# Another hand-written order of four engines around the chunks of a scan that runs beside an MLP

## The reference

```python
mag = np.sqrt(a_re * a_re + a_im * a_im)
scale = np.minimum(mag, 0.999) / (mag + 1e-06)
for t in range(S):
    new_re = ar * S_re - ai * S_im
    new_im = ar * S_im + ai * S_re
    S_re, S_im = (new_re + k[t] outer v[t], new_im)
    y[t] = q[t] @ S_re
h = y @ w_in;  x = (h * clip(h + 3, 0, 6) / 6) @ w_out
h = x @ w2_in; out = (max(h, 0) + alpha * min(h, 0)) @ w2_out
```

## Time and profile before

| | before |
|---|---|
| runs, median (lowest to highest) | 1002.93 us (1001.9 to 1004.77), 3 runs |
| the profiled execution | 1003.23 us |
| its span, first to last instruction | 1001.5 us |
| mean granted clock of PE | 0.998 |
| busy PE, DVE, ACT, POOL | 96%, 58%, 50%, 27% |

### The profile page before, as it was taken

How to read it: one execution, slowest core, us unless ns; L and a number is a source line. 1 busy time by engine, 2 the same in 40 slices (tenths; PEclk the granted TensorE clock), 3 DMA queues, 4 the chain that set the end, 5 groups by cost and what they waited for, 6 DMA issues and landing times.

```text
span 1001.5 us, 17747 instructions
## 1 busy us (share of the span) xinstructions
PE 964.9 (96%) x6858; PEld 868.4 (87%) x6858; DVE 584.1 (58%) x1049; ACT 502.0 (50%) x907; POOL 268.2 (27%) x251
## 2 busy tenths in 40 slices
PE   2899989999999999999999999999999999999998
PEld 2788978999999999999999998888888888888786
DVE  6868886777777767777662345444434444344332
ACT  7767886777777777776643543322222122222111
POOL 0000222222232322322222333332333333323332
PEclk9999999999999999999999999999999999999999
DMA  7853334333444333444320801023060060230000
GB/s 218 216 151 95 96 86 109 94 98 80 111 101 126 95 97 80 108 108 111 88 49 1 308 1 56 0 74 85 1 151 8 0 158 1 68 91 1 32 0 32
DMA packets 86661, 84.72 MB, mean 85 GB/s; under 512 B 31152, under 2 KB 81328, under 8 KB 86192
## 3 DMA queue, kind: packets, MB, share of 16 engines
q1 hardware_dynamic: 86576, 83.58, 31.3%
HBM read 55.10 MB, written 14.19 MB: 69 GB/s over the span
## 4 chain that ended last, share of the span: by engine, by line
PE 82%; ACT 5%; DVE 4%; SPq 3%; DMA 2%; issue 2%; ACTq 0%; DVEq 0%
PE op L1263 12%; PE hp L1264 12%; PE op L1264 11%; PE hp L1263 11%; PE op L1265 11%; PE hp L1265 11%; PE yp L1251 3%; PE gp L1258 2%; PE gp L1230 2%; PE yp L1230 2%; PE hp L1286 2%; PE op L1311 2%; DMA a_sb<-a_in 1%; DMA st<-rows 1%; ACT L608 1%
## 5 line engine op out<-in xcount | busy, mean ns | idle before, releaser
L584 POOL TENSOR_TENSOR g_lo<-gated,g_hi 128x512 fp32r<-128x512 f32 (+2 forms) x240 | 266.0, 1108 | 726.2 <-ACT g_hi L679 726.2
L679 ACT ACTIVATE g_hi<-gated 128x512 fp32r<-128x512 f32 (+2 forms) x240 | 126.3, 526 | 314.7 <-DVE gated L969 273.7
L965 DVE TENSOR_SCALAR gate<-hp,alpha_sb 128x512 f32<-128x512 f32 x96 | 72.0, 750 | 209.5 <-PE hp L1265 209.5
L954 DVE SCALAR_TENSOR_TENSOR gated<-gate,hp 128x256 f32<-128x256 f32 (+1 forms) x160 | 75.2, 470 | 134.1 <-ACT gate L672 133.5
L1263 PE MATMUL op<-g_hi,wb_hi 128*128 128x256 f32 (+1 forms) x432 | 137.5, 318 | 2.3 <-ACT out_sb L684 1.2
L1263 PE MATMUL hp<-x_hi,wa_hi 128*128 128x256 f32 (+1 forms) x432 | 134.8, 312 | 0.3 <-DVE x_lo L918 0.2
L1265 PE MATMUL op<-g_hi,wb_lo 128*128 128x256 f32 (+1 forms) x432 | 132.4, 306 | 0.0
L1264 PE MATMUL hp<-x_lo,wa_hi 128*128 128x256 f32 (+1 forms) x432 | 132.3, 306 | 0.0
L1265 PE MATMUL hp<-x_hi,wa_lo 128*128 128x256 f32 (+1 forms) x432 | 132.3, 306 | 0.0
L1264 PE MATMUL op<-g_lo,wb_hi 128*128 128x256 f32 (+1 forms) x432 | 132.3, 306 | 0.0
L672 ACT ACTIVATE gate<-hp,half 128x256 f32<-128x256 f32 (+1 forms) x160 | 81.2, 507 | 98.7 <-PE hp L1265 89.2
(11 more groups left out here) (115 smaller groups left out, 1652.7 us busy)
## 6 DMA issues: line engine op xcount, KB each, us to landing
st<-prod SPq DMA_DIRECT2D x96, 145.1 KB, 3.0
raw<-a_in SPq DMA_DIRECT2D x4, 2304.0 KB, 15.2
a_sb<-a_in SPq DMA_DIRECT2D x24, 288.0 KB, 3.7
qk_sb<-qk_in SPq DMA_DIRECT2D x24, 288.0 KB, 3.7
rows<-prod SPq DMA_DIRECT2D x48, 96.8 KB, 2.4
st<-rows SPq DMA_DIRECT2D x48, 96.8 KB, 2.8
v_pad<-v_in SPq DMA_DIRECT2D x24, 192.0 KB, 3.5
x_raw<-x SPq DMA_DIRECT2D x6, 768.0 KB, 16.2
```

The costliest lines, as they stand in the source:

```text
L584: pool.tensor_tensor(g_lo[:, at, 0:wide], gated[:, at * UT:at * UT + wide], g_hi[:, at, 0:wide].bitcast(F32), ALU.subtract).then_inc(glo_d ...
L679: act.activation(g_hi[:, at, 0:wide], gated[:, at * UT:at * UT + wide], ACT.Copy).then_inc(ghi_done, 1)
L954: dve.scalar_tensor_tensor(out=gated[:, to], in0=gate[:, at], scalar=1.0, in1=hp[:, n % 2, 0:wide], op0=ALU.min, op1=ALU.mult).then_inc(ga ...
L965: dve.tensor_scalar(gate[:, at], hp[:, n % 2, 0:wide], 0.0, alpha_sb[:, m:m + 1], ALU.min, ALU.mult).then_inc(gate_done, 1)
```

## The change

The strings and `places()` go. Each engine gets a `short_slot` and a `long_slot` in which every step stands where it is to be issued; items over 7 (short) or 5 (long) follow with their own steps only. `due` leaves a step out where there is no such chunk, `if_kept` for a batch's last chunk. `ALONE` and `LENGTHS` differ. A few waits are added that the former order made needless. (SP's calls of `store_due` for the last items of a slot are left out below.)

```diff
-ALONE = 3
-LENGTHS = (6,) + 8 * (7,) + (8, 7, 7, 8) + 2 * (5, 5, 6) + (5, 6, 6)
+PLANNED = {True: 7, False: 5}
+ALONE = 2
+LENGTHS = 6 * (7,) + (8, 7, 7, 8, 8, 7, 7) + 4 * (5,) + (6, 5, 6, 5, 6)
...
@@ SyncE's queue
+    def short_slot(n, c0, c1, c2, c4):
+        due(stack, c1)
+        store_due(n)
+        due(stack_high, c1)
+        due(load_v, c1)
+        store_due(n + 1)
+        due(load_qk, c2)
+        due(load_a, c4)
+        store_due(n + 2)
+    def long_slot(n, c0, c1, c2, c4):
+        due(stack, c1)
+        store_due(n)
+        due(load_qk, c2)
+        due(stack_high, c1)
+        store_due(n + 1)
+        store_due(n + 2)
+        due(load_v, c1)
+        due(load_a, c4)
...
@@ ScalarE
+    def short_slot(n, c0, c1, c2, c3):
+        splits(n)
+        gate_of(n + GSTEP)
+        if_kept(copy_k, c0, 0)
+        high_due(n + GSTEP)
+        leave_due(n)
+        splits(n + 1)
+        gate_of(n + 1 + GSTEP)
+        due(waves, c1)
+        due(copy_ends, c1)
+        if_kept(copy_k, c0, 1)
+        high_due(n + 1 + GSTEP)
+        leave_due(n + 1)
+        splits(n + 2)
+        gate_of(n + 2 + GSTEP)
+        due(logs, c2)
+        high_due(n + 2 + GSTEP)
+        leave_due(n + 2)
+        splits(n + 3)
+        gate_of(n + 3 + GSTEP)
+        due(inverses, c2)
+        high_due(n + 3 + GSTEP)
+        x_high(c0)
+        leave_due(n + 3)
+        splits(n + 4)
+        gate_of(n + 4 + GSTEP)
+        high_due(n + 4 + GSTEP)
+        leave_due(n + 4)
+        splits(n + 5)
+        gate_of(n + 5 + GSTEP)
+        due(squares, c3)
+        high_due(n + 5 + GSTEP)
+        leave_due(n + 5)
+        splits(n + 6)
+        gate_of(n + 6 + GSTEP)
+        due(angle, c2)
+        high_due(n + 6 + GSTEP)
+        leave_due(n + 6)
+    def long_slot(n, c0, c1, c2, c3):
+        gate_of(n + GSTEP)
+        if_kept(copy_k, c0, 0)
+        high_due(n + GSTEP)
+        leave_due(n)
+        gate_of(n + 1 + GSTEP)
+        due(copy_ends, c1)
+        due(waves, c1)
+        due(logs, c2)
+        high_due(n + 1 + GSTEP)
+        leave_due(n + 1)
+        due(squares, c3)
+        x_high(c0)
+        gate_of(n + 2 + GSTEP)
+        due(inverses, c2)
+        high_due(n + 2 + GSTEP)
+        leave_due(n + 2)
+        gate_of(n + 3 + GSTEP)
+        if_kept(copy_k, c0, 1)
+        high_due(n + 3 + GSTEP)
+        leave_due(n + 3)
+        gate_of(n + 4 + GSTEP)
+        due(angle, c2)
+        high_due(n + 4 + GSTEP)
+        leave_due(n + 4)
...
@@ VectorE
     def state(c):
...
+            dve.wait_ge(y_ready, c + 1)
             dve.tensor_tensor(win(s_pad), s_sum[:, :, :], ends, ALU.mult).then_inc(state_ready, 1)
...
+    def short_slot(n, c0, c1, c2, c3):
+        due(phases, c1)
+        gate1(n + GSTEP)
+        due(fractions, c1)
+        mask(c0, 0)
+        splits(n)
+        gate1(n + 1 + GSTEP)
+        due(backward, c1)
+        mask(c0, 1)
+        due(with_qk, c1)
+        splits(n + 1)
+        gate1(n + 2 + GSTEP)
+        due(product, c1, 0)
+        splits(n + 2)
+        due(product, c1, 1)
+        gate1(n + 3 + GSTEP)
+        due(decays, c2)
+        x_low(c0)
+        splits(n + 3)
+        if_kept(state, c0)
+        gate1(n + 4 + GSTEP)
+        due(residue, c2)
+        due(refine, c2)
+        due(ratio, c2)
+        splits(n + 4)
+        gate1(n + 5 + GSTEP)
+        due(mags, c3)
+        splits(n + 5)
+        gate1(n + 6 + GSTEP)
+        due(forward, c2)
+        splits(n + 6)
+    def long_slot(n, c0, c1, c2, c3, led):
+        if not led:
+            due(forward, c1)
+        due(phases, c1)
+        mask(c0, 0)
+        gate1(n + GSTEP)
+        due(fractions, c1)
+        due(backward, c1)
+        mask(c0, 1)
+        gate1(n + 1 + GSTEP)
+        due(with_qk, c1)
+        due(product, c1, 0)
+        due(product, c1, 1)
+        gate1(n + 2 + GSTEP)
+        x_low(c0)
+        gate1(n + 3 + GSTEP)
+        due(residue, c2)
+        due(refine, c2)
+        due(ratio, c2)
+        due(mags, c3)
+        gate1(n + 4 + GSTEP)
+        due(decays, c2)
+        if_kept(state, c0)
...
@@ TensorE
     def turn_k(c, k):
...
+        pe.wait_ge(st_landed[c % 2], 16 * ROWS_DMAS * (c // 2 + 1))
         need(pe, tp_read, 2 * kept(c) + k)
...
     def new_state(c):
         pe.wait_ge(tp_read, 2 * kept(c) + 2)
+        pe.wait_ge(v_landed, 16 * (c + 1))
+        pe.wait_ge(masked, 2 * c + 1)
...
-    for steps, n, c0, c1, c2, c3 in places():
-        keeps = not is_last(c0)
-        if "a" in steps:
-            score(c0, 0)
-            if keeps:
-                turn_k(c0, 0)
-        first_half(n)
-        if "a" in steps:
-            score(c0, 1)
-        second_half(n)
-        if "a" in steps and keeps:
-            turn_k(c0, 1)
-        if "o" in steps:
-            outputs(c0)
-            if keeps:
-                new_state(c0)
+    def short_slot(n, c0):
+        first_half(n)
+        score(c0, 0)
+        if_kept(turn_k, c0, 0)
+        score(c0, 1)
+        second_half(n)
+        if_kept(turn_k, c0, 1)
+        first_half(n + 1)
+        second_half(n + 1)
+        first_half(n + 2)
+        second_half(n + 2)
+        first_half(n + 3)
+        outputs(c0)
+        if_kept(new_state, c0)
+        second_half(n + 3)
+        first_half(n + 4)
+        second_half(n + 4)
+        first_half(n + 5)
+        second_half(n + 5)
+        first_half(n + 6)
+        second_half(n + 6)
+    def long_slot(n, c0):
+        score(c0, 0)
+        if_kept(turn_k, c0, 0)
+        first_half(n)
+        if_kept(turn_k, c0, 1)
+        second_half(n)
+        first_half(n + 1)
+        score(c0, 1)
+        second_half(n + 1)
+        outputs(c0)
+        first_half(n + 2)
+        second_half(n + 2)
+        first_half(n + 3)
+        second_half(n + 3)
+        if_kept(new_state, c0)
+        first_half(n + 4)
+        second_half(n + 4)
+    for items, c0, c1, c2, c3, led in slots():
+        slot = short_slot if is_short(c0) else long_slot
+        slot(items[0], c0)
+        for n in items[PLANNED[slot is short_slot]:]:
+            first_half(n)
+            second_half(n)
```

More of the change, by code:

```diff
@@ L140, in split_count, with slots, due, if_kept @@
     return max(W_ORDER.index(b) for b in blocks) + 1
-def places():
+def slots():
     for s in range(FIRST, NCH):
-        items = items_of(s)
-        plan = (SHORT if is_short(s) else LONG)[len(items)]
-        for steps, n in zip(plan, items):
-            if s > FIRST and is_short(s - 1):
-                steps = steps.replace("B", "")
-            yield (steps, n, chunk_at(s), chunk_at(s + 1),
-                   chunk_at(s + 2), chunk_at(s + 3))
+        yield items_of(s), s, chunk_at(s + 1), chunk_at(s + 2), chunk_at(s + 3), s > FIRST and is_short(s - 1)
+def due(step, c, *what):
+    if c is not None:
+        step(c, *what)
+def if_kept(step, c, *what):
+    if not is_last(c):
+        step(c, *what)
 STORES = [[(max(c, STARTS[u]), min(c + CPU, STARTS[u + 1])) for c in range(0, NCH, CPU)
@@ L743, in _, with splits @@
                     angle(3)
[L745 to L769 removed]
+            def splits(n):
@@ L774, in _ @@
+            for items, c0, c1, c2, c3, led in slots():
+                slot = short_slot if is_short(c0) else long_slot
+                slot(items[0], c0, c1, c2, c3)
+                for n in items[PLANNED[slot is short_slot]:]:
+                    splits(n)
+                    gate_of(n + GSTEP)
+                    high_due(n + GSTEP)
+                    leave_due(n)
             for n in range(N1 - MT_FF, NT):
@@ L924, in state @@
                 if is_first(c):
+                    need(dve, y_ready, c)
                     dve.tensor_tensor(win(s_pad), kv_place(c), ends, ALU.mult).then_inc(state_ready, 1)
@@ L1049, in _ @@
                 gate1(n + GSTEP)
-            for steps, n, c0, c1, c2, c3 in places():
-                if "a" in steps and c1 is not None:
-                    phases(c1)
-                    fractions(c1)
-                    if "B" in steps:
-                        forward(c1)
-                gate1(n + GSTEP)
-                if "c" in steps and c1 is not None:
-                    backward(c1)
-                if "d" in steps and c1 is not None:
-                    with_qk(c1)
-                if "e" in steps and c1 is not None:
-                    product(c1, 0)
-                if "f" in steps:
-                    mask(c0, 0)
-                    mask(c0, 1)
-                if "g" in steps and c1 is not None:
-                    product(c1, 1)
-                if "h" in steps:
-                    x_low(c0)
-                if "i" in steps and not is_last(c0):
-                    state(c0)
-                if "j" in steps and c2 is not None:
-                    residue(c2)
-                    refine(c2)
-                    ratio(c2)
-                if "k" in steps and c2 is not None:
-                    decays(c2)
-                if "l" in steps and c3 is not None:
```

(11 more changed lines are left out.)

60 lines of the change are left out of this document (18 added, 42 removed).

## The result

| | before | after |
|---|---|---|
| runs, median (lowest to highest) | 1003.45 us (1001.9 to 1004.77), 4 runs | 993.12 us (990.54 to 994.13), 4 runs |
| the profiled execution | 1003.23 us | 992.22 us |
| its span | 1001.5 us | 990.2 us |
| mean granted clock of PE | 0.998 | 1.000 |

The ratio is 0.9894, with a 95% interval of 0.9868 to 0.9919. The forecast was 993.6 us, as likeliest of 990.5 to 1001.5. The profiled execution moved by 11.0 us, where the sum had said 9.5.

The account below looks back on a forecast made before the run. TensorE, busy 96% of the span, was taken as the bound, with 10.2 us of waits after 60 us. Terms -6.7 - 1.6 - 1.1 - 0.5 - 1.6 + 0.5 + 1.5 = -9.5 us gave 993.6 us, range 990.5 to 1001.5.

Parts of the forecast that it names:

- Part 2: DVE and ACT order in short slots: second product 3.3 us earlier, all six `st` waits gone, -6.7 us with slow starts.
- Part 1: Short slots' score groups behind half an item: 1.08 us more for `st`, at no cost to PE.
- Part 3: SP order, `load_qk` behind `stack_high` and `load_v` in short slots: only slack, 0; long slots' order as before.
- Part 4: Outputs and state in short slots' fourth item: `scores` waits go, -1.6 us; `x_lo` gain 0.2 offset by 0.2.
- Part 5: ACT's order around POOL: both `g_lo` waits gone, -1.1 us; of the 1.2 us `out_sb` wait 0.7 stays, -0.5.
- Part 6: PE's clock in chunk 6's stretch: 1.6 us lost at the lower level comes back, -1.6 us.
- Part 7: PE's changes between kinds of matmul: short slots -0.5 us, long slots that keep a state +1.0 us; net +0.5.
- Part 9: Chunks 4 and 5, new PE waits for `gated` or `g_lo` in place of `st`: +1.5 us, bounds 0 and 4.
- Part 8: Long slots otherwise: second mask and copy of k come in time; cost 0, bounds 0 and +0.5 us a slot.
- Part 10: `ALONE` 2 and other slot lengths, first slot one f32 item sooner: 0, bounds 0 and +1.5 us.
- Rival A: Chunks 4 and 5: DVE and ACT stay the limit, PE's waits only change name; about 999 us, chance 0.22.
- Rivals B and C: B: long slots' second mask late, 1008 us (0.13); C: new waits, slots 7 to 14, within 3 us of 1003 (0.08).

Follow-up runs that it names:

- act_dve_pair: Changed kernel with everything but ScalarE's and VectorE's lists put back as before (except the first slot's start and length): 1040.28 us, ratio 1.0371.
- act_order_alone: Kernel before, only ScalarE edited: weight splits first in each item, and waves in the second item of short slots: 1012.37 us, ratio 1.0085.

## Why the prediction was right

By its steps, in the traces' terms:

- *Part 2, the two lists: right in what it forecast, too narrow in its reason.* 10.7 us from phases to second product were forecast, 10.65 measured; all six waits for `st` in short slots went. That the two agree to 0.05 us is luck: the phases took 1.73 us instead of 1.22, the first product 0.95 instead of 1.27, and a gate waited 0.15. The step read one slot with splits and let it stand for all six waits; four of them (2.4 of 6.1 us) stood in slots without splits, where only the crossing over `waves` is left. And it described ACT's move as the cure and DVE's as a gate less. DVE's new list alone costs 6.7 us, by its rows because its `x_low` then stands ahead of ACT's `x_high`. The two moves on ACT that the step named cost 7.5 us alone, by the rows because `waves` then stands beside `logs`, whose own move to the third item the step passed over; undone in the changed kernel they cost 5.8. The two whole lists together are all of the short slots' 13 us.
- *Part 1, the late score: named as slack, and that is what it is.* It costs nothing to undo, and alone it gives 2.3 us.
- *Part 3, SP: right for short slots, wrong in its last sentence.* "In long slots SP's order is as before" overlooked `store_due(n)` ahead of `stack_high`. It costs a wait of 1.2 us (1.4 us between the marks), once, in the slot that begins with a unit's last item.
- *Part 4, outputs and masks: -1.8 us (-1.6 as forecast, and the `x_lo` wait's 0.2, against which 0.2 had been set), for the wrong reason.* The outputs' later place is not what did it: put back, it costs nothing. The masks come 3.1 us sooner on DVE besides the score's own move (chunk 4's slot).
- *Part 5:* `g_lo` kept 0.5 of 1.1 us, where all was to go; `out_sb` went whole, where 0.7 was to stay. Together as forecast within 0.2 us.
- *Part 6, the clock: right for the profiled execution.* Granted clock 1.00 from 100 to 190 us; 1.6 us. Two of the four runs of after have a mean clock of 0.998 again, and take 994.0 and 994.1 us; and when `act_dve_pair` was timed, six of seven runs of the kernel before had 1.000 and took 1001.6 to 1002.8 us. So the fall does not come in every execution of the kernel before, and these 1.6 us are partly a matter of which execution was profiled.
- *Part 7, changes between kinds of matmul: mis-sized.* A long slot that keeps a state costs 21.66 against 21.62 us (chunk 19's stretch of before), so 0.04 us and not 0.14; a short slot without waits costs 21.05, where chunk 9's stretch of before took 21.13. In PE's busy time of the two stretches it is +0.5 us (long) and, after the clock's 1.6 us and, by estimate, 0.6 us of slow starts, about -1.4 us (short). The net is -0.9 where +0.5 was set. This term was mis-sized by 1.4 us.
- *Part 9, what comes in place: 1.5 us allowed, nothing came* beyond the `g_lo` already counted. That ACT and DVE are as full as PE in chunks 4 and 5 was read rightly from their busy time, but it does not follow that PE must wait: DVE still stands still nearly as long (46.5 us against 48.0 from 100 to 330 us), only behind the steps that the next score needs.
- *Part 8: right.* No waits for `scores` or `k_rows` in long slots; in chunk 18's slot DVE even waits 1.28 us for the score. But the pair alone shows what PE's new places are worth: with the outputs an item later and `new_state` an item earlier than in the changed kernel, it is 38 us slower than before.
- *Part 10: 0 as set.* The first fp32r matmul starts at 97.08 us instead of 97.36.

Sum of what was measured: -6.7 + 1.3 (chunk 19, with its slow start) - 1.8 - 0.6 - 1.2 - 1.6 - 0.9 = -11.5 us, against 11.0 between the marks and 11.3 in the span. The forecast of 9.5 us was 1.5 short in the profiled execution. It is as near as that because errors cancelled: parts 7 and 9 missed 2.9 us between them one way, and chunk 19's wait 1.3 us the other. The medians moved by 10.3 us, since the profiled run of after lay 0.9 us below its median.

Rival A fell: the idle time of chunks 4 and 5 did not change its name. Rivals B and C did not show: no `scores` wait in the long slots, and nothing new in slots 7 to 14. Shared access shows again, and costs little. DVE's second product in chunk 4's slot starts at 113.52 and takes its 0.94 us; it is POOL that is held up this time, whose subtractions of that size took 0.73 us where nothing met them:

```profile
113.66 1.41 POOL L606 TENSOR_TENSOR g_lo<-gated,g_hi 128x256 fp32r<-128x256 f32 x1 [3.28 <-ACT g_hi L701]
```

That agrees with the rule of the Trainium skill's page "SBUF — State Buffer" (Who interferes with whom) that the one that comes second waits. It is also where PE's last two waits come from, 0.26 us each at 124.57 and 142.37 us: they end with subtractions of 1.14 and 1.12 us, and the first of these started at 123.38, inside DVE's split of 123.24 to 123.92. At 0.73 us neither would have been waited for, by estimate. Over the span POOL is busy 277.1 us instead of 268.2 and DVE 591.5 instead of 584.1.

## What to carry to other kernels

Where two in-order engines feed each other, the list of one can't be judged alone. VectorE's new list in the old kernel lost 6.7 us, two moves out of ScalarE's lost 7.5, and the two whole lists together won 13. By the traces each loss came from a step that stood in one list too early for what it needs from another: `x_low` ahead of `x_high`, the products behind a gate that ACT makes only after `waves` and `logs`, `new_state` ahead of the copy of k. So before such a change is tried, write down for each step that hands over to another engine the item it stands in on both sides, and keep the pairs in step. Whether ScalarE's whole list alone would win or lose is open.

Not all waits count. VectorE waits nearly as long after the change as before it; what was won is that it waits behind the steps on which PE's next score depends. Once the lists match, the place of score and outputs in the short slots is free; in the long slots PE's order has to move with the lists.

## What was not expected of the hardware

The waits of PE in the long slots of `act_dve_pair`, 4.3 us in the mean, brought the granted clock to the lower level again and again: 0.82 to 0.94 in the seven stretches that hold such a wait, 1.00 in chunk 17's, which has none. PE is busy 20.6 us longer for it, so that seven waits of 29.8 us come to 50.4 us, 1.7 times themselves. In the profiled execution of the kernel before, the clock fell once, behind the wait of 1.86 us at chunk 6's score (0.93). The length of one wait does not tell it: in `act_order_alone` PE waits 2.50 us for `out_sb` in chunk 6's stretch, and the clock there is 1.00.
